# Token chunks of 512 instead of 508 in a recurrence followed by a feed-forward layer

## The reference

```python
sig = 1.0 / (1.0 + np.exp(-f_logit))
f = lower_bound + (1.0 - lower_bound) * sig
for t in range(S):
    h = f[:, t] * h + (1.0 - f[:, t]) * x[:, t]
    y[:, t] = h
h = y.reshape(B * S, D) @ w_in
g = np.where(h >= 1, h, np.where(h <= -1, 0.0, (h + 1) ** 2 / 4.0))
out = g @ w_out
```

## Time and profile before

| | |
|---|---|
| median of the runs | 1080.88 us (1079.94 to 1081.30) |
| span of the profiled execution | 1077.3 us, so 3.6 us of the median lie around it |
| PE matmul busy | 1068.0 us, 99% |
| DVE / ACT busy | 804.1 us, 75% / 451.2 us, 42% |
| matmuls | 4,632, of which 4,608 in fp32r: 4,260 of 508 columns, 348 of 492 |
| granted TensorE clock | 1.00 over the whole span |
| DMA | 41.76 MB, 39 GB/s |

### The profile page before, as it was taken

One profiled execution on the slowest core, in us unless ns is written; L12 is line 12 of the kernel. 1 busy time (PEld: TensorE's weight loads), 2 busy tenths in 40 slices (PEclk: granted clock), 3 DMA queues, 4 the chain that ended last, 5 costly groups with the idle time before them and its releaser, 6 DMA issues.

```text
span 1077.3 us, 11996 instructions
## 1 busy us (share of the span) xinstructions
PE 1068.0 (99%) x4632; PEld 868.4 (81%) x4632; DVE 804.1 (75%) x741; ACT 451.2 (42%) x476; POOL 0.2 (0%) x4
## 2 busy tenths in 40 slices
PE   7999999999999999999999999999999999999998
PEld 4788888888888888888888888888888888888887
DVE  7976867778777677786776877868677787776764
ACT  6443444434444344443443434434444344443432
POOL 0000000000000000000000000000000000000000
PEclk9999999999999999999999999999999999999999
DMA  7110101101011010110101101101011010100000
GB/s 272 39 39 20 58 0 58 57 1 58 7 51 58 0 58 19 39 58 0 58 21 37 58 0 58 45 13 58 0 58 58 0 58 14 44 19 1 20 19 19
DMA packets 20010, 41.76 MB, mean 39 GB/s; under 512 B 2336, under 2 KB 15136, under 8 KB 20000
## 3 DMA queue, kind: packets, MB, share of 16 engines
q1 hardware_dynamic: 20000, 41.63, 11.3%
HBM read 29.16 MB, written 12.45 MB: 39 GB/s over the span
## 4 chain that ended last, share of the span: by engine, by line
PE 96%; DVE 3%; DMA 0%; ACT 0%; issue 0%; SPq 0%; DVEq 0%
PE acc L369 16%; PE acc L368 16%; PE h L367 16%; PE acc L367 16%; PE h L369 16%; PE h L368 16%; DVE g L304 1%; DVE g L299 1%; DVE y L287 0%; DMA gate<-f_logit_chunks 0%; DVE g_lo L309 0%; DVE w_out_lo L268 0%; DVE w_in_lo L264 0%; DVE drive L280 0%; DVE gate L273 0%
## 5 line engine op out<-in xcount | busy, mean ns | idle before, releaser
L209 ACT ACTIVATE g<-h 128x1016 f32<-128x1016 f32 (+1 forms) x192 | 195.4, 1018 | 603.8 <-PE h L369 603.8
L299 DVE SCALAR_TENSOR_TENSOR g<-g 128x1016 f32<-128x1016 f32 (+1 forms) x192 | 232.7, 1212 | 259.9 <-ACT g L209 259.9
L367 PE MATMUL h<-y_hi,w_in_lo 128*128 128x508 f32 (+1 forms) x768 | 302.3, 394 | 4.9 <-DVE g L304 2.9
L369 PE MATMUL acc<-g_hi,w_out_hi 128*128 128x508 f32 (+1 forms) x768 | 301.2, 392 | 0.0
L368 PE MATMUL acc<-g_lo,w_out_hi 128*128 128x508 f32 (+1 forms) x768 | 301.1, 392 | 0.0
L369 PE MATMUL h<-y_hi,w_in_hi 128*128 128x508 f32 (+1 forms) x768 | 300.3, 391 | 0.0
L367 PE MATMUL acc<-g_hi,w_out_lo 128*128 128x508 f32 (+1 forms) x768 | 300.3, 391 | 0.0
L368 PE MATMUL h<-y_lo,w_in_hi 128*128 128x508 f32 (+1 forms) x768 | 299.6, 390 | 0.0
L309 DVE TENSOR_TENSOR g_lo<-g,g_hi 128x1016 fp32r<-128x1016 f32 (+1 forms) x192 | 231.7, 1207 | 1.1 <-ACT g_hi L214 1.1
L304 DVE TENSOR_TENSOR g<-g,h 128x1016 f32<-128x1016 f32 (+1 forms) x192 | 230.8, 1202 | 0.0
L214 ACT CAST g_hi<-g 128x1016 fp32r<-128x1016 f32 (+1 forms) x192 | 197.9, 1031 | 7.2 <-DVE g L304 7.2
(11 more groups left out here) (16 smaller groups left out, 82.2 us busy)
## 6 DMA issues: line engine op xcount, KB each, us to landing
gate<-f_logit_chunks SPq DMA_DIRECT2D x48, 254.0 KB, 2.8
drive<-x_chunks SPq DMA_DIRECT2D x48, 254.0 KB, 4.1
out_chunks<-result SPq DMA_DIRECT2D x22, 508.0 KB, 2.7
w_in_f<-w_in_pairs SPq DMA_DIRECT2D x8, 256.0 KB, 5.6
w_out_f<-w_out_pairs SPq DMA_DIRECT2D x8, 256.0 KB, 7.3
out_chunks<-result SPq DMA_DIRECT2D x1, 492.0 KB, 3.8
out_chunks<-result SPq DMA_DIRECT2D x2, 246.0 KB, 2.0
lb<-lower_bound_tiles SPq DMA_DIRECT2D x1, 1.0 KB, 2.4
```

The costliest lines, as they stand in the source:

```text
L209: nc.scalar.activation(g[:, slot, :, 0:width], h[:, h_slot, :, 0:width], ACT.Relu, bias=0.5, scale=0.5).then_inc(t_ready, 1)
L299: nc.vector.scalar_tensor_tensor(out=t, in0=t, scalar=1.0, in1=t, op0=ALU.min, op1=ALU.mult).then_inc(square_ready, 1)
L367: nc.tensor.matmul(dst, w_lo, v_hi, start=start, stop=False)
L369: return nc.tensor.matmul(dst, w_hi, v_hi, start=False, stop=stop)
```

## The change

CHUNK becomes 512, so LAST = 6080 - 11 x 512 = 448. Everything that is sized by CHUNK goes with it: all the buffers named above, the host's padding (12 x 512 = 6,144 tokens in place of 6,096), and the widths of the operations. Numbers of instructions, DMAs and waits stay as they are.

```diff
@@ -26,7 +26,7 @@
 KT = D // P
 PAIRS = FF // (2 * P)
 ROUNDS = 12
-CHUNK = 508
+CHUNK = 512
 LAST = SEQ - (ROUNDS - 1) * CHUNK
 WARM_UP = 24
 BANK = 512
```

## The result

The kernel with chunks of 512 took 1066.4 us (median; 1065.15 to 1068.41, four runs) against 1081.1 us before: ratio 0.986, 95% interval 0.985 to 0.988. It is 1.4% faster; the forecast was 1088.1 us with a range from 1069 to 1092, so both the sign and the range were missed. The profiled execution took 1065.35 us with a span of 1063.4 us, 13.9 us under the 1077.3 of before.

The account below looks back on a forecast made before the run. PE's stream of 4,608 matmuls was taken as the bound. Wide matmuls +13.0 us and narrow ones -5.7 us, together +7.3, with head and tail -0.05, took the median 1080.88 to 1088.1 us; range 1069 to 1092.

Parts of the forecast that it names:

- What bounds the kernel: Whole kernel: it lasts as long as PE's stream of 4,608 matmuls, with PE waiting only 4.8 us, in the first chunk.
- the rest of the spacing: Time between matmul starts beyond columns / 2.4: 18.6 ns for 508 columns; 1 ns of it is 4.6 us.
- head, tail and cover: First chunk before PE starts and end after it: together -0.05 us; DVE's work in chunk 22 hidden, else 0.9 us once.
- That the place of the tiles makes the blocks differ: Blocks of twelve matmuls in chunk 10: 227.5 to 232.5 ns by tile offset to the weights; 2,048-byte tiles give one offset.
- The grid: Matmul starts fall on steps of 6.667 ns, read from two chunks (13,264.0 steps) and one chunk (6,630).
- The pick of 35 steps: Spacing of 512 columns becomes 233.33 ns, 35 steps of 6.667 ns: 4,260 matmuls, +13.0 us; chance 0.42.
- The two groups of the earlier trace: Pair 2's second product, k = 0, before the change: two groups of three passes, 0.68 and 0.70 us, at the coming offset.
- 348 narrow matmuls with the same rest as the wide: Last round's 448-column matmuls: 206.67 ns each, where 492 columns took 223.03; -5.7 us.
- The offset modulo 128: Moving tiles' places counted in stretches of 128 bytes; after the change all start 64 bytes past a multiple of 128.
- 1,728 columns more: 36 matmuls issued at full width for the last round work on 64 columns too many, not 16: +0.72 us.
- the rest at its mean: First rival, matmul stream: spacing beyond columns / 2.4 stays 18.6 ns, one offset or eight; 1081.5 us, chance 0.17.
- The fast pattern: Second rival, matmul stream: alternating 34 and 35 steps, 230.0 ns for 512 columns, 203.3 for 448; -8.1 us, chance 0.31.

Follow-up runs that it names:

- PE alone: Kernel without the layer, PE running only stretches of 36 matmuls, other engines idle; 512 columns at 64 bytes took 228.9 ns five times, 233.3 once.
- the one execution of 1065.24 us: One execution, without trace, of the kernel before with its 508-column tiles in buffers 512 wide; six others took 1075.9 to 1078.7 us, median of seven 1077.55.

## Why the prediction was wrong

**What bounds the kernel, and that the rest of the spacing is the term to size**: right. Waits, head, tail and cover moved by tenths of a us, and no PE wait on DVE came in chunk 22.

**That the place of the tiles makes the blocks differ, and that equal places make them alike**: right, and shown from both sides: by unequal places at the new widths (1080.55 us), and by three other common places (1058.6, 1083.0, 1087.4 us) with the same widths.

**The grid**: right in kind. Settled patterns of three or seven matmuls add up to whole steps of 6.667 ns (102, 103, 105; 241, 244). But I allowed only whole steps for one matmul, or two in turn; 34 1/3 was not on my list. Of the two sums that I gave for the grid, the one over a single chunk shows nothing, since a start is read to 10 ns and a step is 6.667.

**The pick of 35 steps**: this is the step that failed. The term 4,260 x (233.33 - 230.28) = +13.0 us was -5.9 us, with 228.89 ns in place of 233.33: 18.9 of the 21.7 us by which the forecast was off. The pick rested on the mean rest of the kernel before, 18.6 ns, rounded up to the grid. It was thin by its own terms: half way between the values 230.0 and 233.33 is 231.67 ns, a rest of 18.3 (not 18.0), so 0.3 ns decided the sign. And that mean says nothing of a common place: over the sixteen distances the settled rest runs from 13.3 to 21.3 ns for 512 columns, and 64 bytes happens to have 15.6. The two groups of the earlier trace rows, which I took for the coming place, had 227 and 233 ns, and I chose by the mean rather than leave it even. PE alone has two values there too, 228.9 five times and 233.3 once; all eight executions of the kernel after have times of the first.

**348 narrow matmuls with the same rest as the wide**: wrong. 448 columns have 13.3 ns at this place and 512 have 15.6. Of the 6.7 ns that each had too much in the sum, 4.4 come from the pick and the others from this step. The term was -5.7 us in the sum and measured -8.0.

**The offset modulo 128**: wrong, it is modulo 256, and between weights and tiles. For the place after the change it was harmless, since 64 bytes is 64 by either. For the evidence it was not: by the sizes of the buffers the low parts g_lo of the groups in the earlier trace rows lay at 192 modulo 256 and only g_hi at 64, so no group of three passes in the kernel before lay as all of them do after.

**1,728 columns more**: they can't be told from the rest in the time. Taking back the 36 x 64 columns, with the tiles at 256 bytes, gave 0.82 us where 0.86 was worked out, so such columns cost what others do. It was the smallest of the terms that count.

**The rivals**: the rest at its mean (1081.5 us) fell, with rests of 15.6 and 13.3 ns. The fast pattern, with 0.31, had the sign and was the nearest, at 1072.8 us for 1066.4, though its turns of 34 and 35 steps aren't the pattern that came. The range stopped 2.6 us short: its low end gave all 4,608 the rest of the shortest block, 15.8 ns. The wide matmuls went 0.3 ns further, 1.2 us, and the narrow ones 2.5 ns, 0.9 us; the rest is the 0.5 us between the change of the spans and that of the medians.

What stays open: why the distance acts as it does. The runs tie it to fp32r (bf16 has none of it), to the width, and to the distance from weights to moving tile modulo 256; what in the engine makes a matmul wait was not tried. What picks one of two patterns, why weights at odd multiples of 16 bytes have other values, and the one execution of 1065.24 us are open too. Why the kernel of before has just 230.28 ns in its mixture wasn't rebuilt either.

## What to carry to other kernels

Where a stream of fp32r matmuls is the bound, read its spacing to a fraction of a ns over thousands of matmuls, and subtract columns / 2.4: here 1 ns is 4.6 us, and moving all tiles by 32 to 192 bytes with one unused buffer changed the kernel by 29 us (1058.6 to 1087.4) with nothing else touched. A common place isn't better by itself: with chunks of 512, unequal places gave 1080.6 us, common ones 1058.6 to 1087.4. But it makes the spacing something that one can choose. Give all moving tiles one distance to the weights (a tile stride that is a multiple of 256 bytes; 2,048 here), then try a few distances on the chip, for each width that the kernel uses; a change of tile width or buffer size moves it by accident, in either direction. A mean over mixed places can't tell which value a common place will have.

## What the runs showed of the hardware

With the weights at multiples of 128 bytes, the spacing of fp32r matmuls of one shape at full clock (2.4 GHz) depends on the distance in bytes from the weights to the moving tile, modulo 256: 226.7 to 234.7 ns for 512 columns, 200.0 to 206.7 for 448, with PE alone at work. With weights at multiples of 32 bytes it did so too in all cases but one; with weights at odd multiples of 16 the values were others (230.0 ns at distance 0 where they were 226.7). The streams of the kernels with a common place repeat patterns of three, five or seven matmuls that add up to whole steps of 6.667 ns, which is 64 bytes of a moving tile at that clock: 103 steps for three of 512 columns, 152 for five of 448 (202.7 ns), 244 for seven of 512. One set of instructions and places can settle in more than one pattern: 228.9 or 233.3 ns for 512 columns at 64 bytes, after different beginnings. bf16 matmuls of 512 columns took 215.8 ns at all eight places tried. After a wait of PE of 2.75 us the granted clock was 0.50 for 3.4 us, with fp32r matmuls of 512 columns 427 ns apart, where they are 227 to 235 at full clock; the trace with a wait of 1.81 us has the full clock there.
